# Retention attention with two feed-forward stages: per-head matmuls in halves of the TensorE array, 2 KB rows, and a later zero fill

## The reference

```python
# attention: B, H, S, DH = 4, 8, 576, 64
scores = q @ k.T / sqrt(DH)
Dmat   = where(rel >= 0, gamma[h] ** rel, 0)   # rel = query position - key position
out    = (scores * Dmat) @ v                    # no softmax
# feed-forward on x (2304 x 512):  softplus(x @ w_in) @ w_out,   d_ff = 2048
# top-2 of 8 experts per token:    sum_k w_k * (relu(x @ w1[e]) @ w2[e]),   d_ff = 1024
```

## Time and profile before

| | us |
|---|---|
| median of 3 runs (lowest, highest) | 1109.94 (1108.17, 1111.71) |
| profiled execution: span from first to last instruction (no other time of it is given) | 1108.1 |
| TensorE busy | 1068.9 (96%) |
| VectorE / ScalarE / GpSimd busy | 403.6 / 429.8 / 237.7 |

### The profile page before, as it was taken

One profiled execution on the slowest core, in us unless ns is written; L12 is line 12 of the kernel. 1 busy time (PEld: TensorE's weight loads), 2 busy tenths in 40 slices (PEclk: granted clock), 3 DMA queues, 4 the chain that ended last, 5 costly groups with the idle time before them and its releaser, 6 DMA issues.

```text
span 1108.1 us, 21819 instructions
## 1 busy us (share of the span) xinstructions
PE 1068.9 (96%) x5723; PEld 928.5 (84%) x5724; DVE 403.6 (36%) x758; ACT 429.8 (39%) x731; POOL 237.7 (21%) x212
## 2 busy tenths in 40 slices
PE   8999999999999999999748999999999999999997
PEld 6999999999999999999636888888888888888885
DVE  2544345234243342432652533654321224222211
ACT  1222366455454554545612533645222223222221
POOL 4443000002002020020741123223222222222222
PEclk9988999999999999999968999999999999999999
DMA  9876111001000000040312552664422121212111
GB/s 249 249 209 195 39 57 57 29 1 29 0 0 29 0 7 22 0 158 24 129 53 66 192 177 86 233 230 168 140 76 66 53 66 50 76 48 66 50 52 41
DMA packets 71266, 96.19 MB, mean 87 GB/s; under 512 B 40622, under 2 KB 51246, under 8 KB 67121
## 3 DMA queue, kind: packets, MB, share of 16 engines
q1 hardware_dynamic: 48560, 67.32, 19.1%
q0 software_dynamic: 11152, 28.37, 8.1%
q10 hardware_dynamic: 11520, 0.09, 0.6%
HBM read 79.98 MB, written 20.37 MB: 91 GB/s over the span
## 4 chain that ended last, share of the span: by engine, by line
PE 91%; DVE 2%; DMA 2%; issue 2%; ACT 1%; POOL 1%; ACTq 1%; SPq 0%; DVEq 0%; POOLq 0%
PE bank L581 25%; PE bank L583 24%; PE bank L582 24%; PE bank L724 3%; PE bank L525 3%; PE bank L539 2%; PE bank L699 2%; PE bank L540 2%; PE bank L543 2%; PE bank L552 1%; PE bank L636 1%; PE bank L513 1%; PE bank L630 1%; DVE g_lo L1054 1%; POOL lists L432 0%
## 5 line engine op out<-in xcount | busy, mean ns | idle before, releaser
L581 PE MATMUL bank<-ew,hT_hi 128*128 x328 | 131.8, 402 | 2.2 <-DVE hT_lo L1257 2.2
L581 PE MATMUL bank<-ew,xgT_hi 128*128 (+1 forms) x328 | 131.7, 402 | 0.0
L583 PE MATMUL bank<-xs_hi,mw 128*128 (+1 forms) x384 | 130.3, 339 | 0.0
L581 PE MATMUL bank<-xs_hi,mw 128*128 (+1 forms) x384 | 130.1, 339 | 0.0
L582 PE MATMUL bank<-xs_lo,mw 128*128 (+1 forms) x384 | 129.6, 337 | 0.0
L583 PE MATMUL bank<-ew,xgT_lo 128*128 (+1 forms) x328 | 128.4, 391 | 0.0
L583 PE MATMUL bank<-ew,hT_lo 128*128 x328 | 128.3, 391 | 0.0
L582 PE MATMUL bank<-ew,hT_hi 128*128 x328 | 127.8, 390 | 0.0
L582 PE MATMUL bank<-ew,xgT_hi 128*128 (+1 forms) x328 | 127.7, 389 | 0.0
L581 PE MATMUL bank<-mw,g_hi 128*128 128x512 f32 x288 | 116.7, 405 | 5.7 <-DVE g_lo L1054 5.7
L432 POOL DMA_INDIRECT lists<-rec,slot x36 | 35.0, 973 | 371.8 <-DVE slot L1142 362.7
(11 more groups left out here) (155 smaller groups left out, 1867.4 us busy)
## 6 DMA issues: line engine op xcount, KB each, us to landing
raw<-w_ex SPq DMA_DIRECT2D x32, 1024.0 KB, 4.9
stage<-w_ff SPq DMA_DIRECT2D x16, 512.0 KB, 4.2
out<-zero SPq DMA_DIRECT2D x3, 1536.0 KB, 8.7
x_rows<-x2sb SPq DMA_DIRECT2D x6, 768.0 KB, 4.2
kbuf<-kN SPq DMA_DIRECT2D x16, 256.0 KB, 3.3
qbuf<-qT SPq DMA_DIRECT2D x16, 256.0 KB, 4.5
vbuf<-vN SPq DMA_DIRECT2D x32, 128.0 KB, 4.0
qdec<-c_q SPq DMA_DIRECT2D x4, 256.0 KB, 4.6
```

The lines of the kernel that those rows point to most:

```text
L581: pe.matmul(o, a_hi, b_hi, start=first, stop=False)
L583: return pe.matmul(o, a_lo, b_hi, start=False, stop=last)
```

## The change

- `scores` alternates between the even and the odd head of a pair, so consecutive matmuls use array rows 0 to 63 and 64 to 127 in turn.
- `output` does the four state matmuls of a chunk first, then eight v matmuls, each of which loads 64 columns of v and writes its head's 64 rows of PSUM (one column half of the array). The zero-padded v buffer becomes a plain one; GpSimd's memset of the padding goes.
- `add_state` makes 8 products of 64 x 64 instead of 4 of 128 x 128.
- q and its table are laid out by chunk on the host, so that a load has one row of 2 KB per partition (4 pairs x 128 x 4 bytes); v comes in one DMA with 2 KB rows instead of two with 256 byte rows.
- The identity is loaded alone ahead of the transposes, the rest of `square` later.
- The zero fill of `out` is taken out of the batch loop. It is issued as three DMAs after the last weight piece, from a tile of its own (`blank`) with 1 KB rows, and ScalarE's wait for it ahead of the feed-forward goes.

The number of records on TensorE stays the same in scores and output, and doubles in the state update.

```diff
             def load_v(b, t):
                 r = ROWS[t]
-                src = vN[bass.ds(b * S + t * P, r), :].rearrange("r (h e d) -> r h e d", e=2, d=DH)
-                for e in range(2):
-                    sp.dma_start(vbuf[0:r, t, :, 3 * e, :], src[:, :, e, :]).then_inc(ld_v[t], 16)
+                sp.dma_start(vbuf[0:r, t, :], vN[bass.ds(b * S + t * P, r), :]).then_inc(ld_v[t], 16)
...
-            sp.dma_start(square[:, :, :], c_sq[:, 0:3, :]).then_inc(ld_mask, 16)
+            sp.dma_start(square[:, 0, :], c_sq[:, 0, :]).then_inc(ld_ident, 16)
...
-
-                part = N // (B - 1)
-                sp.dma_start(out[bass.ds((b - 1) * part, part), :].rearrange("(t p) n -> p t n", p=P),
-                             spread(zero[:, :], 1, [P, part // P, D])).then_inc(ld_zero, 16)
             for f in range(2 * B, FT1):
                 sp.wait_ge(piece_lo, f - 1)
                 load_piece(f, f % 2)
+            sp.wait_ge(blanked, 1)
+            part = N // (B - 1)
+            for i in range(B - 1):
+                sp.dma_start(out[i * part:(i + 1) * part, :].rearrange("(p t) (u n) -> p (t u) n", p=P, u=2),
+                             spread(blank[:, :], 1, [P, 2 * part // P, D // 2])).then_inc(ld_zero, 16)
...
-            pool.memset(vbuf[:, :, :, 1:3, :], 0.0).then_inc(cleared, 1)
-            pool.wait_ge(cleared, 3)
+            pool.memset(blank[:, :], 0.0).then_inc(blanked, 1)
...
-                for e in range(2):
-                    for h in range(PAIRS):
-                        last = pe.matmul(sc_ps[e][0:r, h, 0:r], kTb[e * DH:(e + 1) * DH, t % 3, h, 0:r],
-                                         qbuf[e * DH:(e + 1) * DH, t, h, 0:r], start=True, stop=True)
-                    last.then_inc(scores_made, 1)
+                q = q_of(t)
+                for h in range(PAIRS):
+                    for e in range(2):
+                        d = slice(e * DH, (e + 1) * DH)
+                        last = pe.matmul(sc_ps[e][0:r, h, 0:r], kTb[d, t % 3, h, 0:r], q[d, h, :],
+                                         start=True, stop=True)
+                        if h == PAIRS - 1:
+                            last.then_inc(scores_made, 1)
...
+                    q = q_of(t)
+                    for h in range(PAIRS):
+                        pe.matmul(x_ps[:, h, 0:r], state[:, (t - 1) % 2, h, :], q[:, h, :],
+                                  start=(h == 0), stop=False, skip_group_check=True)
                 for h in range(PAIRS):
-                    o = x_ps[:, h, 0:r]
-                    pe.matmul(o, vbuf[0:r, t, h, 0:2, :], sco[0:r, t % 3, 0, h, 0:r], start=True, stop=False)
-                    last = pe.matmul(o, vbuf[0:r, t, h, 2:4, :], sco[0:r, t % 3, 1, h, 0:r],
-                                     start=False, stop=(t == 0))
-                    if t:
-                        last = pe.matmul(o, state[:, (t - 1) % 2, h, :], qbuf[:, t, h, 0:r],
-                                         start=False, stop=True)
+                    for e in range(2):
+                        last = pe.matmul(x_ps[e * DH:(e + 1) * DH, h, 0:r],
+                                         vbuf[0:r, t, (2 * h + e) * DH:(2 * h + e + 1) * DH],
+                                         sco[0:r, t % 3, e, h, 0:r], start=(t == 0 and h == 0), stop=True,
+                                         skip_group_check=True)
...
                 for h in range(PAIRS):
-                    last = pe.matmul(kv_ps[:, h, :], kbuf[:, t, h * P:(h + 1) * P],
-                                     vbuf[:, t, h, 0:4:3, :], start=True, stop=True)
+                    for e in range(2):
+                        d = slice((2 * h + e) * DH, (2 * h + e + 1) * DH)
+                        last = pe.matmul(kv_ps[e * DH:(e + 1) * DH, h, 0:DH], kbuf[:, t, d], vbuf[:, t, d],
+                                         start=True, stop=True)
...
             act.wait_ge(scaled, 2 * B * CHUNKS)
-            act.wait_ge(ld_zero, 16 * (B - 1))
             act.wait_ge(scores_masked, 2 * B * CHUNKS)
```

More of the change, by code:

```diff
@@ L52, with by_chunk @@
 PAD_TOKEN = N
+def by_chunk(a):
+    parts = [a[:, :, :, t * P:t * P + r].transpose(0, 2, 1, 3).reshape(len(a), P, PAIRS * r)
+             for t, r in enumerate(ROWS)]
+    return np.ascontiguousarray(np.concatenate(parts, axis=2))
 def table_consts():
@@ L60, in table_consts @@
     kdec = gamma[:, None] ** (-pos[None, :])
-    q = np.repeat(qdec, DH, axis=0).reshape(PAIRS, P, S).transpose(1, 0, 2)
+    q = by_chunk(np.repeat(qdec, DH, axis=0).reshape(1, PAIRS, P, S))[0]
     k = np.zeros((CHUNKS * P, H))
@@ L106, in build @@
         kbuf, a = place("kbuf", [P, CHUNKS, D], F32, R_W2)
-        vbuf, a = place("vbuf", [P, CHUNKS, PAIRS, 4, DH], F32, a)
-        qbuf, a = place("qbuf", [P, CHUNKS, PAIRS, P], F32, a)
+        vbuf, a = place("vbuf", [P, CHUNKS, D], F32, a)
+        qbuf, a = place("qbuf", [P, CHUNKS, D], F32, a)
         kTb, a = place("kTb", [P, 3, PAIRS, P], F32, a)
@@ L122, in build @@
         x2T, R_C = place("x2T", [P, KT, P], F32, a)
-        qdec, a = place("qdec", [P, PAIRS, S], F32, R_T + 3 * KT * TOK * 4)
+        qdec, a = place("qdec", [P, PAIRS * S], F32, R_T + 3 * KT * TOK * 4)
         kdec, a = place("kdec", [P, CHUNKS, H], F32, a)
@@ L164, in build @@
         pick, a = place("pick", [P, 2, TJ, E], F32, a)
+        blank, a = place("blank", [P, D // 2], F32, a)
         tab, a = place("tab", [1, 9, MAX_TILES], I32, R_X + 32768)
@@ L208, in build @@
         ld_small, ld_kdec, ld_mask, ld_zero = (sem(n) for n in ("ld_small", "ld_kdec", "ld_mask", "ld_zero"))
+        ld_ident, blanked = sem("ld_ident"), sem("blanked")
         ld_lists, passed = sem("ld_lists"), sem("passed")
@@ L261, in as32, with q_of @@
             return ap.bitcast(F32)
+        def q_of(t):
+            return qbuf[:, t, 0:PAIRS * ROWS[t]].rearrange("p (h s) -> p h s", h=PAIRS)
         def spread(ap, axis, shape):
@@ L286, in load_q @@
                 r = ROWS[t]
-                sp.dma_start(qbuf[:, t, :, 0:r],
-                             qT[bass.ds(b, 1), :, :, t * P:t * P + r].rearrange("o h p s -> p (o h) s")
+                sp.dma_start(qbuf[:, t, 0:PAIRS * r],
+                             qT[bass.ds(b, 1), :, t * D:t * D + PAIRS * r].rearrange("o p n -> (o p) n")
                              ).then_inc(ld_q[t], 16)
@@ L292, in load_v @@
                 r = ROWS[t]
-                src = vN[bass.ds(b * S + t * P, r), :].rearrange("r (h e d) -> r h e d", e=2, d=DH)
-                for e in range(2):
-                    sp.dma_start(vbuf[0:r, t, :, 3 * e, :], src[:, :, e, :]).then_inc(ld_v[t], 16)
+                sp.dma_start(vbuf[0:r, t, :], vN[bass.ds(b * S + t * P, r), :]).then_inc(ld_v[t], 16)
             def load_qdec(t):
-                c = slice(t * P, t * P + ROWS[t])
-                sp.dma_start(qdec[:, :, c], c_q[:, :, c]).then_inc(ld_qdec[t], 16)
+                c = slice(t * D, t * D + PAIRS * ROWS[t])
+                sp.dma_start(qdec[:, c], c_q[:, c]).then_inc(ld_qdec[t], 16)
             def load_piece(f, i):
@@ L318, in _ @@
             load_piece(1, 1)
+            sp.dma_start(square[:, 1:3, :], c_sq[:, 1:3, :]).then_inc(ld_small, 16)
             sp.dma_start(small[:, :], c_small[:, 0:104]).then_inc(ld_small, 16)
@@ L420, in _ @@
                                        ).then_inc(scaled, 1)
-                    q = qbuf[:, t, :, 0:r]
+                    q = qbuf[:, t, 0:PAIRS * r]
                     pool.wait_ge(ld_qdec[t], 16)
@@ L424, in _ @@
                     pool.wait_ge(scaled, (b * CHUNKS + t) * 2 + 1)
-                    pool.tensor_tensor(q, q, qdec[:, :, t * P:t * P + r], ALU.mult).then_inc(scaled, 1)
+                    pool.tensor_tensor(q, q, qdec[:, t * D:t * D + PAIRS * r], ALU.mult).then_inc(scaled, 1)
             def send_records(c):
@@ L503, in _ @@
                 pe.matmul(gate_ps[:, :], zero[:, 0:P], zero[:, :], start=True, stop=True)
-            pe.wait_ge(ld_mask, 32)
-            pe.wait_ge(cleared, 3)
+            pe.wait_ge(ld_ident, 16)
+            pe.wait_ge(cleared, 2)
             def transpose_k(b, t):
@@ L532, in output @@
                 pe.wait_ge(scores_masked, n * 2 + 2)
-                alone(pe, ld_v[t], b * 32 + 32)
+                alone(pe, ld_v[t], b * 16 + 16)
                 at_least(pe, x_kept, n)
@@ L671, in _ @@
             ff_in(0, 1)
-            pe.wait_ge(ld_small, 48)
+            pe.wait_ge(ld_small, 64)
             ff_chunk(0, False, True)
@@ L1005, in add_state @@
                         last = dve.tensor_tensor(state[p, t % 2, :, p], state[p, (t - 1) % 2, :, p],
-                                                 kv_ps[p, :, p], ALU.add)
+                                                 kv_ps[p, :, 0:DH], ALU.add)
                     else:
-                        last = dve.tensor_copy(state[p, 0, :, p], kv_ps[p, :, p])
+                        last = dve.tensor_copy(state[p, 0, :, p], kv_ps[p, :, 0:DH])
```

(8 more changed lines are left out.)

## The result

| | before | after |
|---|---|---|
| median of 4 runs (lowest, highest), us | 1110.08 (1108.17, 1111.71) | 1072.84 (1070.54, 1076.79) |
| profiled execution: its time, span | not given, 1108.1 | 1076.79, 1074.9 |
| TensorE busy | 1068.9 | 1029.2 |

The ratio is 0.966, with a 95% interval of 0.963 to 0.969; 1071 us was forecast. The profiled execution is the slowest of the four. On the page TensorE keeps 96% of the span; the chain's share of TensorE falls from 91% to 86%.

A forecast was written before the change was run, and what follows sets the result against it. TensorE was taken as the bound, with DMA bounding the first batch. First batch 8, three batches 25, last output 2 and clock 4 sum to 39 us off the 1108.1 us span: 1069, as a median 1071 us, range 1061 to 1090.

The forecast's parts named there:

- Scores: Attention scores of a full chunk: alternating row halves makes 16 records take 0.97 us, shape change included, instead of 1.64.
- Column halves: Attention output: 16 v records in two column halves running at once take 0.89 us, instead of 1.78 in series.
- rival B: v and update records: column halves' loads are not hidden, 0.167 us a v record; 1125 us, chance 0.06.
- Rivals A: Attention: only row halves overlap, column halves go in series; 23.4 us a batch, 1087 us, chance 0.15.
- E: Attention: alternation does nothing in rows or columns; only shape changes and some of the first batch gain; 1101 us, chance 0.03.
- Shape changes: Changing the array's shape on TensorE in attention costs 0.14 us a change at most.
- A batch: An attention batch takes 18.4 us, 8.4 less than now; three batches at full clock give 25 us.
- Who is late next: Batch boundary: VectorE frees chunk 0's banks some 0.2 us after TensorE asks for them.
- The first batch: Bound by DMA; with larger rows at 3.1 us a chunk it ends at 27.8 instead of 35.75 us, 8 us gained.
- Clock: Falls to half clock, twice in attention and once after, cost 7.8 us; 4 us of it was taken as gained.
- Rival C: Attention: the clock takes half-array work for rest and stays at 1.2 GHz; 1131 us, chance 0.04.
- Rival D: Attention: another engine or the DMA holds a batch at 21.8 us; 1085 us, chance 0.05.

The follow-up runs named there:

- scores_grouped: The changed kernel, but scores do the four even heads first, then the four odd ones; 1082.18 us, ratio 0.973 to the kernel before.
- v_grouped: The changed kernel, but a chunk's v matmuls do the four even heads (left column half) first, then the odd ones; 1083.21 us, ratio 0.973 to the kernel before.
- The repeat: The changed kernel measured again with no edit; 1075.62 us, ratio 0.968 to the kernel before.
- state_between: The changed kernel, but each pair's state matmul stands directly ahead of its two v matmuls; 1088.0 us, ratio 0.977 to the kernel before.
- small_rows: The changed kernel, but q and its table come in 512 byte rows and v in two DMAs of 256 byte rows; 1082.37 us, ratio 0.973.
- zero_early: The changed kernel, but the zero fill of out is back in the batch loop, from its own tile; 1078.97 us, ratio 0.971 to the kernel before.
- pe_part_alone: The changed kernel with the small q, table and v rows and the zero fill back in the batch loop; 1090.54 us, ratio 0.981 to the kernel before.

## Why the prediction was right

- **Scores** (0.97 us): 1.09. The mechanism is shown by scores_grouped. My 0.102 us a record was itself a mean over overlapping records: of the grouped scores at 56.69 us in scores_grouped, at most three are under way in a slice of 0.11 us near either end, and up to six in the middle, where even heads give way to odd ones.
- **Column halves** (0.89 for 16 v records, no row of before): 1.02 with the change of shape in it; v_grouped shows the overlap. That is 0.064 us a record, where rival B and the rule behind it ask for 0.167: here the loads of column halves are hidden. Rivals A, B and E fall.
- **Update** (0.60, bounds 0.45 and 0.89): 0.46. **64-row scores** (0.65): 0.61 with the change in it. The doubt about density was unfounded.
- **Shape changes** (0.14 at most): 0.17, and a chunk has four, of which the sum had priced one at 0.09 and two at 0.14. The row may have hidden part of the price: its records stream 64 columns, and I counted them at 0.111 us; in the changed kernel eight state matmul records take 54.52 - 53.48 = 1.04 us with 64 columns and 1.09 with 128. This under-sized term makes the chunk 4.26 instead of 4.07 us; the two dense terms give some back.
- **A batch** (18.4 us): 18.68 and 18.58 in the third and fourth, 22.10 in the second, of which 2.0 are a wait for masks and 1.7 half clock.
- **Who is late next** (0.2 us at the boundary): 0.18 in the third and fourth batch, but 2.0 in the second, which I had not followed. "TensorE waiting for masks" was one of the signs that I had named against the prediction; it came in one batch of three and cost little. There the first batch's order puts a piece, a split of x and the mask in a row. The timeline of VectorE, and GpSimd's beside it:

```profile
30.93 1.76 DVE L1030 TENSOR_TENSOR mw<-stage,mw 128x1024 fp32r<-128x1024 f32 x1 [0.26 <-ACT mw L840]
32.61 1.62 DVE L1052 TENSOR_TENSOR xs_lo<-xT,xs_hi 128x384 fp32r<-128x384 f32 x1
34.26 1.29 DVE L1012 TENSOR_TENSOR sco<-bank,mask 128x512 f32<-128x512 f32 x2
```

```profile
30.56 1.04 POOL L431 TENSOR_TENSOR kbuf<-kbuf,kdec 128x512 f32<-128x512 f32 x1
31.68 2.13 POOL L437 TENSOR_TENSOR qbuf<-qbuf,qdec 128x512 f32<-128x512 f32 x1
33.89 1.24 POOL L431 TENSOR_TENSOR kbuf<-kbuf,kdec 128x512 f32<-128x512 f32 x1
```

- **The first batch** (8 us, end at 27.8): 6.1, end at 29.70. The size of one term was wrong: 1.05 MB in 3.1 us a chunk is 339 GB/s, above both of my rates (276 and 336) and not between them. DMA moved 311 GB/s, and GpSimd's q products of chunks 0 to 3 start from 7.37 to 17.43 us, 3.35 us apart. So k of the second batch, though issued at 17.47 us and not at 20, is scaled at 24.75 rather than 23, and this is nearly all of the 1.9 us.
- **The last output** (2 us): 2. **Zeroing** (nothing in the feed-forward): nothing shown; three issues at 139.4 us, the next store at 163.02, and the feed-forward's 3.8 us are accounted for without it.
- **Clock** (4 of 7.8 us): the half-clock stretches fell from 17.0 us in three to 3.4 in one, so 6.8 us. Windows of TensorE alone (busy, clock, DMA share, GB/s), right behind the 2.0 us wait:

```profile
36.90:40.30 3.40, 3.40 (x36) 0.50 0.63 167
```

  The repeat fell at the same place; the two kernels with a shorter wait there (scores_grouped, 1.2 us) or none (state_between) had no fall. In small_rows, zero_early and pe_part_alone, too, each fall begins in or soon behind a wait of 1.1 to 3.8 us, but the changed kernel's wait of 2.10 us ahead of 13.65 us has none behind it. That the wait causes the fall is argued, not shown. Rival C falls.
- **Rival D** fails for the change (DMA work 0.77 x 18.68 = 14.4 us a batch; 16.3 was my upper count) but holds in pe_part_alone: against its 21.8 us a batch stand 24.2 and 22.2 us of DMA work, and batches of 25.2 and 24.1.

The sum again, with half clock taken out of the batches on both sides: the first batch gave 6.1 us (8 forecast), the other three 6.5, 8.2 and 7.6, together 22.3 (25), the last output 2.1 (2), the clock 6.8 (4): 37.3 where 39 was forecast and the medians say 37.2. The mechanisms are right one by one. That the total is right to 2 us is in part luck: the four batches fell 4.6 us short, and the clock, for which I had taken the middle between nothing and all, gave 2.8 back.

## What to carry to other kernels

Small-head attention fills TensorE with half-used arrays; let consecutive matmuls alternate between two row halves or two column halves, and keep all work of one array shape together, at 0.17 us a change. Look in the old trace for places where two halves met by accident: here they priced the new order. And count what the faster engine will ask of DMA: here the TensorE part alone ran into it (0.981), and only with larger rows and the fill moved away came 0.966.

## What was not expected of the hardware

- TensorE looks ahead over matmuls of the other array half: in v_grouped the update's first records, for the left half, started at 52.77 us, while v records for the right half that come before them in the program started until 53.09.
- VectorE and GpSimd slow each other. The split of x takes 0.56 us where GpSimd is idle (the kernel before, below) and 1.62 above; GpSimd's q product takes 2.13 instead of 1.27. The Trainium skill, "SBUF — State Buffer", Who interferes with whom, says that the two share a port pair under an exclusive lock, and that a VectorE instruction with two SBUF inputs contends there with a GpSimd instruction that reads SBUF; this case's rows agree, as both got longer. That such meetings are part of what made masks late is argued, not shown.

```profile
69.78 0.56 DVE L1034 TENSOR_TENSOR xs_lo<-xT,xs_hi  x1 [3.34 <-ACT xs_hi L804]
```

- The expert stage varies by itself: 551.4 us in one execution of the changed kernel (523.5 to the end of the span, 1074.9) and 547.0 in another (523.4 to 1070.4). Differences of a few us are read from the stage, not from the total.
